# Turning Mixture's result between two layers: TensorE's transposes and ScalarE's copies replaced by VectorE's 32 by 32 blocks and transfers over DRAM

## The reference

```
x   = attention(q, k, v)                 # 8 heads of 64, causal window of 128, ALiBi bias
P   = exp(x @ w_gate - max);  8 rounds:  P /= P.sum(1);  P /= P.sum(0);  P *= N / E
x2  = sum over 8 experts e of  P[:, e] * (relu(x @ w1[e]) @ w2[e])     # "Mixture", hidden 1024
out = leaky(x2 @ w_in) @ w_out           # leaky(h) = max(0.01 h, h), hidden 2048
```

## Time and profile before

| | |
|---|---|
| median of 3 runs | 2050.15 us |
| the profiled execution | 2049.61 us, its span 2047.8 us |
| TensorE matmuls, busy | 2032.2 us, 99% |
| VectorE, busy | 1183.9 us, 58% |
| ScalarE, busy | 643.1 us, 31% |
| GpSimd, busy | 1167.4 us, 57% |
| mean DMA rate | 51 GB/s |
| granted TensorE clock | 0.999 of full speed |

### The profile page before, as it was taken

The page is one execution under the profiler, slowest core; times in us unless marked ns, Lnnn a source line. Parts: engine busy times, 40 slices in busy tenths (PEclk is TensorE's granted clock), DMA queues, the critical chain, the costliest instruction groups (busy, mean ns, idle before and its releaser), DMA issues.

```text
span 2047.8 us, 36400 instructions
## 1 busy us (share of the span) xinstructions
PE 2032.2 (99%) x12475; PEld 1815.3 (89%) x12475; DVE 1183.9 (58%) x2708; ACT 643.1 (31%) x1776; POOL 1167.4 (57%) x1451
## 2 busy tenths in 40 slices
PE   8999999999999999999999999999999999999999
PEld 6788999899999899999999999999999989998998
DVE  8876766555555555564555554554554565667666
ACT  8972222222222222233222222222222244334332
POOL 3425556555566565576555566655555575667551
PEclk9999999999999999999999999999999999999999
DMA  5311111111111111111111111111111111111211
GB/s 178 119 66 42 42 42 41 51 41 51 41 41 41 51 41 51 41 37 47 42 52 41 51 41 41 41 51 41 51 41 41 41 41 52 42 52 56 73 42 47
DMA packets 31311, 104.86 MB, mean 51 GB/s; under 512 B 3968, under 2 KB 4480, under 8 KB 31232
## 3 DMA queue, kind: packets, MB, share of 16 engines
q1 hardware_dynamic: 31232, 103.84, 15.1%
HBM read 99.11 MB, written 4.72 MB: 51 GB/s over the span
## 4 chain that ended last, share of the span: by engine, by line
PE 95%; DVE 2%; POOL 1%; ACT 1%; issue 1%; DMA 0%; SPq 0%; ACTq 0%; DVEq 0%; POOLq 0%
PE bank L1227 16%; PE bank L1228 16%; PE bank L1229 16%; PE bank L1205 14%; PE bank L1208 14%; PE bank L1207 14%; PE bank L1146 1%; PE bank L1124 1%; PE bank L1116 1%; PE bank L1159 1%; ACT sc L541 1%; DVE sc L792 1%; POOL up_lo L369 0%; DVE sc L776 0%; PE bank L1243 0%
## 5 line engine op out<-in xcount | busy, mean ns | idle before, releaser
L876 DVE SCALAR_TENSOR_TENSOR acc<-bank,gate,acc 128x512 f32<-128x512 f32 x495 | 371.6, 751 | 573.8 <-PE bank L1229 573.8
L1205 PE MATMUL bank<-x_hi,up_hi 128*128 128x256 f32 (+1 forms) x2240 | 663.3, 296 | 2.0 <-POOL up_lo L369 1.9
L1208 PE MATMUL bank<-x_hi,up_lo 128*128 128x256 f32 (+1 forms) x2240 | 662.9, 296 | 0.0
L1207 PE MATMUL bank<-x_lo,up_hi 128*128 128x256 f32 (+1 forms) x2240 | 662.3, 296 | 0.0
L1228 PE MATMUL bank<-down_lo,hs_hi 128*128 128x512 f32 x1440 | 568.0, 394 | 0.0
L1227 PE MATMUL bank<-down_hi,hs_hi 128*128 128x512 f32 x1440 | 567.5, 394 | 0.4 <-DVE hs_lo L990 0.4
L1229 PE MATMUL bank<-down_hi,hs_lo 128*128 128x512 f32 x1440 | 560.3, 389 | 0.0
L1205 PEld LDWEIGHTS bank<-x_hi,up_hi 128*128 128x128 f32 x2240 | 423.9, 189 | 30.0 <-POOL up_lo L369 2.7
L1207 PEld LDWEIGHTS bank<-x_lo,up_hi 128*128 128x128 f32 x2240 | 423.9, 189 | 23.6
L1208 PEld LDWEIGHTS bank<-x_hi,up_lo 128*128 128x128 f32 x2240 | 423.8, 189 | 0.0
L369 POOL TENSOR_TENSOR up_lo<-stage_up,up_hi 128x256 fp32r<-128x256 f32 x546 | 384.7, 742 | 6.3
(11 more groups left out here) (118 smaller groups left out, 1823.1 us busy)
## 6 DMA issues: line engine op xcount, KB each, us to landing
stage_up<-w_up SPq DMA_DIRECT2D x80, 512.0 KB, 3.4
stage_down<-w_down SPq DMA_DIRECT2D x80, 512.0 KB, 3.4
qk<-qk SPq DMA_DIRECT2D x15, 608.0 KB, 3.8
v_nat<-v SPq DMA_DIRECT2D x16, 320.0 KB, 2.9
result<-acc SPq DMA_DIRECT2D x16, 256.0 KB, 2.6
result<-acc SPq DMA_DIRECT2D x4, 128.0 KB, 3.0
qk<-qk SPq DMA_DIRECT2D x2, 128.0 KB, 2.1
qk<-qk SPq DMA_DIRECT2D x1, 192.0 KB, 2.5
```

The costliest lines, as they stand in the source:

```text
L876: last = d.scalar_tensor_tensor(out=to, in0=y[:, :], scalar=share(g, tile, e), in1=to, op0=ALU.mult, op1=ALU.add)
L1205: m.matmul(to[:, 0:n], up_hi[s][:, w], x_hi[u][:, x], start=first and c == 0, stop=False, skip_group_check=True)
L1207: m.matmul(to[:, 0:n], up_hi[s][:, w], x_lo[u][:, x], start=False, stop=False, skip_group_check=True)
L1208: last = m.matmul(to[:, 0:n], up_lo[s][:, w], x_hi[u][:, x], start=False, stop=c == 1, skip_group_check=True)
```

## The change

TensorE's `transpose_x2` and ScalarE's `copy_x2` go. In their place:

- VectorE transposes each tile of the accumulator (128 by 512) in blocks of 32 by 32 into one of two new SBUF buffers, `x2_turned`, at the same two points of a unit: behind the results of tiles 1 and 3 (`turn_x2`). Before it writes a buffer again it waits until the stores from it have landed (`x2_out`).
- ScalarE, where it copied, now issues four stores per tile (`send_x2`), one for each 32 partitions, into a scratch tensor `x2_mem` in DRAM. They put the blocks in their places; a piece is 32 numbers, 128 bytes, and a store has 512 of them.
- In the next unit, behind the copies of `t1` and `t5` and ahead of that of `u2`, ScalarE waits for the stores of the two tiles of the unit before and issues the loads into `xr` (`fetch_x2`), one per tile, two for tile 6. GpSimd and ScalarE wait for the loads (`x2_in`) where they first read `xr`.
- VectorE's program has granules 34 and 35 written out instead of looped.

```diff
+            def send_x2(n):
+                act.wait_ge(x2_tr, n + 1)
+                to = x2_mem[n, :, :].rearrange("(r d) (k a t) -> r d k a t", d=32, k=KD, a=4)
+                for quad in range(4):
+                    part = x2_turned[n % 2][quad * 32:quad * 32 + 32, :].rearrange("d (k r t) -> d k r t", k=KD, r=4)
+                    act.dma_start(to[:, :, :, quad, :].rearrange("r d k t -> d k r t"), part).then_inc(x2_out[n % 2], 16)
+            def fetch_x2(n):
+                act.wait_ge(x2_out[n % 2], 64 * (n // 2 + 1))
...
+                src = x2_mem[n, :, :].rearrange("p (k t) -> p k t", k=KD)
                 for half, t, cols, p0 in token_parts(n % TILES):
                     to = xr[:, half * HALF:(half + 1) * HALF].rearrange("p (k t) -> p k t", t=S)[:, :, t:t + cols]
-                    last = a.activation(to, src[:, :, p0:p0 + cols], ACT.Copy)
-                last.then_inc(x2_copied, 1)
+                    act.dma_start(to, src[:, :, p0:p0 + cols]).then_inc(x2_in, 16)
...
+            def turn_x2(k, point):                      # VectorE
...
+                for n in x2_tiles(k // 2, k % 2)[point:point + 1]:
+                    g, tile = n // TILES, n % TILES
+                    if tile == 0:
+                        dve.wait_ge(y_free, TILES * (G1, F0)[g])
+                    if n > 1:
+                        dve.wait_ge(x2_out[n % 2], 64 * (n // 2))
+                    d.transpose(x2_turned[n % 2][:, :], acc[g][:, tile * D:(tile + 1) * D]).then_inc(x2_tr, 1)
...
-            def transpose_x2(n):                        # TensorE
...
-                for kd in range(KD):
-                    c = tile * D + kd * P
-                    last = m.transpose(b_m[:, kd * P:(kd + 1) * P], acc[g][:, c:c + P], ident[:, :])
-                last.then_inc(x2_tr, 1)
```

More of the change, by code:

```diff
@@ L3, with attention_moe_ffn @@
 from contextlib import ExitStack
-def attention_moe_ffn(nc, qk_t, v_t, w_gate, w_up, w_down, out, shape):
+def attention_moe_ffn(nc, qk_t, v_t, w_gate, w_up, w_down, out, x2_mem, shape):
     fp32, f32r = mybir.dt.float32, mybir.dt.float32r
@@ L85, in attention_moe_ffn @@
         t1, t5, u2 = (place(n, NU[1]) for n in ("t1", "t5", "u2"))
+        x2_turned = [place(f"x2_turned{n}", D) for n in range(2)]
         ident = place("ident", P)
@@ L157, in attention_moe_ffn @@
         g_done, leak_done = sem("g_done"), sem("leak_done")
-        x2_tr, x2_copied, stored = (sem(n) for n in ("x2_tr", "x2_copied", "stored"))
+        x2_tr, x2_in, stored = (sem(n) for n in ("x2_tr", "x2_in", "stored"))
+        x2_out = [sem(f"x2_out{n}") for n in range(2)]
         def rows_of(g):
@@ L500, in take_sum @@
                     else:
-                        pool.wait_ge(x2_copied, TILES * (phase - 1))
+                        pool.wait_ge(x2_in, 16 * (TILES + 1) * (phase - 1))
                 if j in (1, 2):
@@ L603, in casts @@
                         act.wait_ge(a_done, 4 * k)
+                    if phase > 1 and u == 0:
+                        act.wait_ge(x2_in, 16 * (TILES + 1) * (phase - 1))
                     cast(A11, x_quarter(phase, 0, 0, u))
@@ L646, in copy_x2, with unit @@
                     act.wait_ge(x_low, 4 * turn_of(n // TILES + 1, 1))
-                src = b_m[:, :].rearrange("p (k t) -> p k t", t=P)
+                src = x2_mem[n, :, :].rearrange("p (k t) -> p k t", k=KD)
                 for half, t, cols, p0 in token_parts(n % TILES):
                     to = xr[:, half * HALF:(half + 1) * HALF].rearrange("p (k t) -> p k t", t=S)[:, :, t:t + cols]
-                    last = a.activation(to, src[:, :, p0:p0 + cols], ACT.Copy)
-                last.then_inc(x2_copied, 1)
-            def unit(k, u, x2=(), phase=None):
+                    act.dma_start(to, src[:, :, p0:p0 + cols]).then_inc(x2_in, 16)
+            def unit(k, u, x2=(), x2_before=(), phase=None):
                 n = NU[u]
                 early_copies(k, u)
+                for tile in x2_before:
+                    fetch_x2(tile)
                 casts(phase, k, 0)
@@ L662, in unit @@
                 for tile in x2[0:1]:
-                    copy_x2(tile)
+                    send_x2(tile)
                 act.wait_ge(c22_done, k + 1)
@@ L672, in unit, with leaky_unit @@
                 for tile in x2[1:2]:
-                    copy_x2(tile)
-            def leaky_unit(k, u, x2=(), phase=None):
+                    send_x2(tile)
+            def leaky_unit(k, u, x2=(), x2_before=(), phase=None):
                 n = NU[u]
@@ L742, in turn @@
                     for u in range(2):
[L743 removed]
+                        next_unit(2 * m + u, u, x2_tiles(m, u), x2_tiles(m - 1 + u, 1 - u))
             turn(G1, unit, unit)
@@ L990, in plain_low @@
                 d.tensor_tensor(hs_lo[u][:, part], of[:, 0:NU[u]], hs_hi[u][:, part], ALU.subtract).then_inc(lo_done, 1)
+            def turn_x2(k, point):
+                if not isinstance(k, int):
+                    return
+                for n in x2_tiles(k // 2, k % 2)[point:point + 1]:
[5 more added lines that the diff above has]
+                    d.transpose(x2_turned[n % 2][:, :], acc[g][:, tile * D:(tile + 1) * D]).then_inc(x2_tr, 1)
             def unit(k, u, prev):
@@ L1011, in unit @@
                 tile(1)
+                turn_x2(k, 0)
                 low(k, u, 1, 0, 0, b_b)
@@ L1024, in unit @@
                 tile(3)
+                turn_x2(k, 1)
                 if u == 0:
@@ L1090, in _ @@
                 pair(j, 0)
-            for n in range(G1 - 2, G1 + 2):
+            for n in range(G1 - 2, G1 + 4):
                 granule(n)
-            with dve.Fori(G1 // 2 + 1, F0 // 2 - 1) as j:
+            with dve.Fori(G1 // 2 + 2, F0 // 2 - 1) as j:
                 pair(j, 1)
@@ L1274, in operand_ready, with unit @@
                     pe.wait_ge(x_low, 4 * (turn - 1) + min(n, 3) + 1)
-            def unit(k, u, s, prev, x2=()):
+            def unit(k, u, s, prev):
                 a_bank, c_bank = b_a[u], b_c[u]
@@ L1311, in unit @@
                 gating(k, 1)
-                for n in x2[0:1]:
-                    transpose_x2(n)
                 pe.wait_ge(t5_copied, k + 1)
@@ L1331, in unit @@
                     tile(4)
-                for n in x2[1:2]:
-                    transpose_x2(n)
             def granule(n):
-                unit(2 * n, 0, n % 2, (n - 1, (n - 1) % 2) if n else None, x2_tiles(n, 0))
-                unit(2 * n + 1, 1, n % 2, (n, n % 2), x2_tiles(n, 1))
+                unit(2 * n, 0, n % 2, (n - 1, (n - 1) % 2) if n else None)
+                unit(2 * n + 1, 1, n % 2, (n, n % 2))
             def pair(j):
@@ L1398 @@
     out = nc.dram_tensor("result", (b * s, h * d), mb.dt.float32, kind="ExternalOutput").ap()
-    attention_moe_ffn(nc, *args, out, (b, h, s, d))
+    x2_mem = nc.dram_tensor("x2_mem", (2 * ((b * s + 255) // 256), 128, 512), mb.dt.float32, kind="Internal").ap()
+    attention_moe_ffn(nc, *args, out, x2_mem, (b, h, s, d))
     r = run_bass_kernel_spmd(nc, [arrays], core_ids=[0])
```

6 lines of the change are left out of this document (removed).

## The result

The changed kernel takes 2057.84 us, median of 7 runs (2056.3 to 2059.94), the kernel before 2050.32 (median of 7 beside it). The ratio is 1.0039, 95% interval [1.0029, 1.0048]: 7.5 us slower, where 8.8 were forecast. A second set gave 2057.91 against 2050.24, ratio 1.0041 [1.0028, 1.0055].

What follows compares the result with a forecast made beforehand. TensorE, busy 99% of the span, was taken to bound the kernel. Waits of 16.8 us lost less 8.0 won made 8.8 more: 2049.6 + 8.8 = 2058.4, 2059 as median; forecast's own range 2051 to 2073, whole range 2045.5 to 2079.

Steps and rivals of the forecast that it cites:

- The gain, 8.0: Removing TensorE's transposes after a tile's last down matmul saves 0.45 us per tile, 18 tiles: 8.0 us.
- VectorE's transpose, 0.6, free: Each of VectorE's 18 SBUF-to-SBUF transposes of 128x512 takes 0.6 us, taken from between 0.35 and 1.34.
- An issue of 0.61: A store issue holds ScalarE's queue 0.61 us: 0.33 plain plus 0.71 - 0.43 for cutting into pieces; 2.65 per tile's four.
- The landing, 2.5: A tile's stores land 2.5 us after the last issue; ScalarE waits for that before issuing loads.
- Rival 2: Small-piece stores land 3.9 us later than assumed, lengthening each of eight waits before `u2`: 30 more, 2089 us; chance 0.13.
- Mixture unit 1 into 0: End stores delay `t1`, so TensorE waits 1.3 before S2, and 0.4 for `u2`: 1.7 at two places, 3.4 us.
- Leaky unit 1 into 0: Stores inside the ScalarE-VectorE relay: waits 0.7 before S1, 2.75 for `t1`, 0.65 for `u2`; 4.1 twice, 8.2 us.
- Leaky unit 0 into 1: Second low part in time; TensorE waits 1.55 for `t1` and 0.4 for `u2`: 1.95 twice, 3.9 us.
- Sum 16.8: Forecast total of TensorE's waits: 3.4 Mixture, 8.2 and 3.9 leaky, 1.3 for tile 6's extra load.
- landed, then the loads are issued, 1.3, then `u2`: Between `t5` and `u2`, ScalarE waits for the last stores, then issues two loads taking 1.3 us, before copying `u2`.
- tile 6's third load: Tile 6 has one load more ahead of `u2`, costing 0.66 twice: 1.3 us.
- Mixture unit 0 into 1: `t1` wanted at 5.4, comes 5.15; `u2` wanted at 8.54, comes 8.35: no wait, cover only 0.2 us.

Runs made afterwards that it cites:

- `no_transfers`: Changed kernel without stores, loads and their waits, ScalarE copying the turned buffer to `xr` (values not the layer's): 2042.93 us, ratio 0.9961 to the kernel before.
- `vector_added`: Kernel before with only VectorE's 18 transposes added, into buffers nothing reads: 2050.28 us against 2050.72, ratio 0.9997.
- `wide_pieces`: Changed kernel with each tile's four stores in 32 pieces of 2 KB instead of 512 of 128 bytes (block positions wrong): 2046.64 us, ratio 0.998.
- `loads_late`: Changed kernel with the loads issued one unit later, same place between `t5` and `u2`: 2057.04 us, ratio 1.0039; run again 2056.54 beside the changed kernel's 2057.91.

## Why the prediction was right, step by step

- **The gain, 8.0.** 7.8 in the runs of `no_transfers`, 7.9 in the stretches of its trace. (18 times 0.45 is 8.1; the forecast wrote 8.0.)
- **VectorE's transpose, 0.6, free.** 0.70, and free (`vector_added`).
- **An issue of 0.61 in the middle of 0.33 and 0.71.** 0.65 for the stores and 0.57 for the loads. The share that comes from cutting a transfer into pieces was the right thing to take from the row of the gate's weights in the earlier trace rows. This number decided the sign: with 0.44 (`wide_pieces`) the change is a gain of 4.
- **The landing, 2.5.** Median 2.2 in both traces, up to 4.7. Rival 2, small written pieces, did not happen: in the 5 us from 944 to 949 of the changed kernel 2112 packets took 30.3% of 16 engines, which is 24.2 us or 0.0115 us each. The Trainium skill's 512 bytes ("DMA: Bandwidth & Descriptors", "Specifications") are a rule on the rate; a piece of 128 bytes was cheap here, and the rate is not what this kernel waits for.
- **The Trainium skill's rule that starting a DMA usually takes little beside the DMA itself** (same page, "Issuing engines are not separate DMA queues"). For one store the trace has 0.65 beside a landing of 2.2; the four in a row, 2.65, take longer than a landing. In front of a copy that TensorE waits for they were most of the loss, and moving all issues to another queue was worth 15 us.
- **The waits by place**, forecast against the first and the second trace. Mixture unit 1 into 0, before S2: 1.3 at each of two against 1.60 and 1.22 in both. Leaky unit 1 into 0, before S2: 2.75 against 2.21 and 1.91, and 2.21 and 2.23; before S1: 0.7 against 1.46 and 0, and 1.39 and 0.66. Leaky unit 0 into 1, before S2: 1.55 against 1.23 and 1.19, and 1.20 and 0.56; before S3: 0.4 against 0.33 and 1.78, and nothing. Sum 16.8 against 15.8 and 12.9.
- **What was wrong in it: the step "landed, then the loads are issued, 1.3, then `u2`".** No wait stood before S3 behind a unit 1, where 0.4 and 0.65 were forecast, nor for tile 6's third load (1.3 in all). The timeline above shows why: the load of the middle tile, landed long ago, is issued at 947.41 while ScalarE still copies `t1` and `t5`, for its queue runs ahead of its engine; so one issue follows the landing and not two. The terms, 3.4 in the sum, have to come off.
- **What was not in it: Mixture unit 0 into 1**, forecast at nothing with a cover of 0.2. In granule 33 it had 0.19 before S2, in granule 34 it had 1.16 before S2 and 1.47 before S3 (0.87 and 0.76 in the second trace), where in the first trace four stores took 3.70 instead of 2.65 and the last of them landed after 4.7 instead of 2.2 (last section). The thin cover was named, but priced at zero.
- **What was luck.** The last two errors nearly cancel in the first trace (3.4 too much, 2.8 too little). In the second the waits less the gain make 4.9 us, and it is mostly a lower clock, which the forecast did not have, that brings the stretches to 7.0. So the order of the queue and the price of an issue were right; that the sum came within 1.3 us of the result is in part chance.

## What to carry to other kernels

When one engine is busy for 99% and others feed it, price a change by what stands in order ahead of each result that the busy engine waits for; total busy time of the feeding engine says little. A DMA issue held its queue for 0.33 to 0.65 us here, longest where the transfer is cut into 512 pieces, and belongs on a queue that nobody waits for. Before believing one trace on a wait that hangs on a landing, take another.

## What the runs showed of the hardware that was not expected

**Issues that fell together with an instruction load were 1 us longer.** In the first trace of the changed kernel 14 of the 18 groups of four stores took 2.62 to 2.74 us, but one 3.70 at 957 and one 3.86 at 1702, where a single issue of the four took 1.73 and 1.85. From 957.6 to 959.4 the DMA queues, and the four issues:

```profile
q10 hardware_dynamic: 513, 0.06, 22.0%
q8 instruction: 1, 0.02, 4.7%
```
```profile
957.12 3.70 ACTq L650 DMA_DIRECT2D x_mem<-x_turned  x4
...
960.91 0.58 ACTq L662 DMA_DIRECT2D xr<-x_mem  x1
964.85 0.56 ACTq L662 DMA_DIRECT2D xr<-x_mem  x1
```

In the four traces of the changed kernel and `loads_late` seven groups of four took over 3.3 us. All seven hold a packet of an "instruction" queue, and none of the 14 short ones of the first trace does. It is not the whole story: in both traces of `loads_late` one issue near 979 took 1.1 to 1.2 us with no such packet. That the load of instructions holds up the issue was not tried.

**Landings beside a weight load were late.** The last store before 960.91 landed only by 964.85, 4.7 us after its issue; SyncE had issued a weight load of 512 KB at 960.48. The other landing of 4.7, of the store issued at 1725.86, has one at 1726.16. In the first trace the 17 stores issued from 0.35 us before to 2 us after a weight load landed after 2.9 to 4.7 us, median 3.5; the other 55 have a median of 2.2, and 12 of them took 2.5 to 3.6. That the weight load is the cause was not tried.

**Waits of TensorE can cost more than they last.** In the second trace of the changed kernel the stretches differ from the kernel before by 0.8 and 6.2, 7.0 in sum, but waits less gain make 12.9 - 8.0 = 4.9. Most of the rest is the clock. Windows of that trace (columns: stretch, length, busy time of PE, PEld, DVE, ACT and POOL, then granted clock, DMA share, GB/s):

```profile
1708.00:1711.00 3.00, 0.99 (x8) 0.79 (x7) 1.36 (x3) 0.67 (x3) 3.00 (x5) 1.00 0.41 72
1711.00:1714.00 3.00, 3.00 (x14) 2.47 (x13) 0.18 (x2) 0.66 (x2) 1.02 (x2) 0.64 0.62 154
1714.00:1717.00 3.00, 3.00 (x17) 2.79 (x17) 2.57 (x6) 0.39 (x1) 0.00 (x0) 0.79 0.59 213
1717.00:1720.00 3.00, 3.00 (x17) 2.59 (x16) 1.92 (x5) 1.41 (x5) 0.00 (x0) 1.00 0.50 86
```

Behind a wait of 1.39 at 1705.6 and one of 2.21 at 1710.7 the grant fell to the lower of the two levels (1.2 of 2.4 GHz) for a while: a matmul of 512 columns followed the one before by 0.43 us instead of 0.23. By the two windows that costs an estimated 3 x 0.36 + 3 x 0.21 = 1.7 us. The second trace of `loads_late` has the same (0.59 and 0.85 in the same two windows). The first traces of both, with the same waits of 2.2 in the same place, do not, and neither does the second trace of the changed kernel behind its wait of 2.23 at 1739.3. So a wait of this size is not enough, and what decides is not shown. It is a price that the forecast did not have.
